# A recurrence followed by two MLPs on one core: later weight loads, two inverses one behind the other, and identity products in TensorE's waits

## What is computed

```python
for t in range(S):
    y[:, :, t] = np.einsum('bhd,bhde->bhe', rt, state)
    Sa = np.einsum('bhde,bhe->bhd', state, at)
    state_decay = state * wt[:, :, None, :] - np.einsum('bhd,bhe->bhde', Sa, bt)
    state = state_decay + np.einsum('bhd,bhe->bhde', vt, kt)
...
h = x @ w_in                                   # 320 x 2048
x = np.maximum(0.01 * h, h) @ w_out            # 2048 x 320
gate = 1.0 / (1.0 + np.exp(-(x @ w_gate)))     # 320 x 1536
out = (gate * (x @ w_val)) @ w_out2            # 1536 x 320
```

## Time and profile before

| | us |
|---|---|
| median of three runs | 1167.99 |
| lowest and highest | 1159.88, 1174.42 |
| the profiled execution | 1176.43 |
| its span, first to last instruction | 1174.7 |

### The profile page before, as it was taken

How to read it: one execution, slowest core, us unless ns; L and a number is a source line. 1 busy time by engine, 2 the same in 40 slices (tenths; PEclk the granted TensorE clock), 3 DMA queues, 4 the chain that set the end, 5 groups by cost and what they waited for, 6 DMA issues and landing times.

```text
span 1174.7 us, 35939 instructions
## 1 busy us (share of the span) xinstructions
PE 1061.2 (90%) x15840; PEld 905.7 (77%) x15840; DVE 596.3 (51%) x1307; ACT 397.6 (34%) x782; POOL 109.4 (9%) x100
## 2 busy tenths in 40 slices
PE   3476595888999999989999999999999999999998
PEld 3476474776878787877778787888888888888887
DVE  8674674796667865666756232443323232322322
ACT  2323232333443533343344334553322222222322
POOL 7201102022020202020200000000000000000000
PEclk9996698988999998989999999999999999999999
DMA  5836215536353533444351205330010102020000
GB/s 174 260 70 217 57 29 142 130 93 172 85 139 87 165 84 107 114 131 94 105 140 51 70 8 170 102 93 23 15 45 1 59 1 59 1 59 1 23 1 23
DMA packets 134985, 99.79 MB, mean 85 GB/s; under 512 B 96560, under 2 KB 111920, under 8 KB 134832
## 3 DMA queue, kind: packets, MB, share of 16 engines
q1 hardware_dynamic: 132384, 85.06, 27.2%
q0 software_dynamic: 2448, 12.45, 3.0%
HBM read 78.61 MB, written 18.87 MB: 83 GB/s over the span
## 4 chain that ended last, share of the span: by engine, by line
PE 75%; DVE 9%; issue 8%; DMA 3%; ACT 2%; POOL 1%; SPq 1%; ACTq 0%; DVEq 0%; POOLq 0%
PE pair_low L866 12%; PE pair L919 11%; PE pair_low L919 6%; PE bank L919 6%; DVE prod L1402 3%; PE bank L939 3%; PE bank L938 3%; PE bank L937 3%; DVE t_unit L1406 2%; PE bank L840 2%; PE bank L831 2%; PE pair_low L883 2%; PE pair_low L884 1%; PE pair_low L885 1%; PE bank L883 1%
## 5 line engine op out<-in xcount | busy, mean ns | idle before, releaser
L1452 DVE TENSOR_TENSOR g_lo<-g_full,g_hi 128x512 fp32r<-128x512 f32 x168 | 122.7, 730 | 237.1 <-ACT g_hi L1167 237.0
L1167 ACT CAST g_hi<-g_full 128x512 fp32r<-128x512 f32 x168 | 104.4, 621 | 134.7 <-DVE g_full L1504 131.6
L866 PE MATMUL pair_low<-x_hi,w_up 128*128 128x512 f32 x440 | 131.8, 432 | 6.2 <-ACT x_hi L1176 3.4
L1160 ACT ACTIVATE g_full<-pair_low 128x512 f32<-128x512 f32 x88 | 52.7, 599 | 211.3 <-PE pair_low L866 198.6
L1402 DVE TENSOR_TENSOR prod<-t_unit,p_unit 128x126 f32<-128x126 f32 (+22 forms) x341 | 93.9, 275 | 24.8 <-DMA p_unit<-p_dram 14.6
L1406 DVE TENSOR_TENSOR t_unit<-t_unit,prod 128x126 f32<-128x126 f32 (+22 forms) x341 | 96.7, 284 | 11.7
L866 PEld LDWEIGHTS pair_low<-x_hi,w_up 128*128 128x128 f32 x440 | 82.3, 200 | 25.8 <-ACT x_hi L1176 3.5
L1504 DVE TENSOR_TENSOR g_full<-pair,h_sb 128x512 f32<-128x512 f32 x36 | 24.9, 691 | 112.8 <-PE pair L919 112.0
L866 PE MATMUL pair_low<-x_lo,w_up 128*128 128x512 f32 x264 | 78.4, 407 | 0.0
L1504 DVE TENSOR_TENSOR g_full<-bank,h_sb 128x512 f32<-128x512 f32 x36 | 24.9, 691 | 94.7 <-PE bank L919 86.3
L383 POOL TENSOR_TENSOR k_sb<-k_sb,inv 128x512 f32<-128x512 f32 x24 | 32.5, 1360 | 368.0 <-DMA k_sb<-in_kF 368.0
(11 more groups left out here) (232 smaller groups left out, 2564.4 us busy)
## 6 DMA issues: line engine op xcount, KB each, us to landing
b_sb<-in_bF SPq DMA_DIRECT2D x12, 512.0 KB, 6.3
a_sb<-in_aF SPq DMA_DIRECT2D x24, 256.0 KB, 6.4
k_sb<-in_kF SPq DMA_DIRECT2D x12, 512.0 KB, 5.0
v_sb<-in_vF SPq DMA_DIRECT2D x12, 512.0 KB, 6.7
r_sb<-in_rF SPq DMA_DIRECT2D x12, 512.0 KB, 8.6
p_unit<-p_dram SPq DMA_DIRECT2D x22, 256.0 KB, 4.1
w_raw<-in_wF SPq DMA_DIRECT2D x20, 260.0 KB, 3.6
stage<-in_w_out POOLq DMA_DIRECT2D x7, 640.0 KB, 7.2
```

The costliest lines, as they stand in the source:

```text
L866: last = nc.tensor.matmul(up_bank(m)[:], lhs, rhs, start=(e == 0), stop=(e == len(products) - 1))
L1160: nc.scalar.activation(g_full[:], up_bank(m)[:], ACT.Lrelu).then_inc(g_ready, 1)
L1167: nc.scalar.copy(g_hi[:, m % 2], g_full[:]).then_inc(g_hi_ready, 1)
L1452: nc.vector.tensor_tensor(g_lo[:, m % 2], g_full[:], g_hi[:, m % 2].bitcast(F32), ALU.subtract).then_inc(g_lo_ready, 1)
```

## The change

Five things are changed, all in the start and in stages of unit 2.

1. POOL asks for the first weights after T of unit 0 has landed (`t_loaded` at 64) and no longer after P of unit 0 has; its b, a and k of units 0, 1 and 2 all stand ahead of the weights, and k 0 and 1 behind b and a of halves 2 and 3.
2. DVE does the scans of halves 0 to 5 first, then the inverses of units 0 and 1 one behind the other. The masked copies `ka` 0 to 3, which stood between scans and inverses, now stand inside the inverses, behind column 18. To allow it, scans 0 to 2 have places for `inv` of their own (`spare_d`, laid over `w_dn1`), and raw decays of halves 4 and 5 use places of `w_first`.
3. `fill` puts products of the identity with itself (128 x 128) into TensorE's list: 24 at the beginning, 10 before the first `first`, and two or three at eight later places.
4. The state ahead of unit 0 is zero, so `sn` and `y_begin` of halves 0 and 1 are gone. `kb` 2 and 3 stand ahead of `first` 2 and 3, `kb` 4 and 5 inside the first MLP steps. ACT does `act_a` 4 and 5 behind `u` and `ut` of halves 0 and 1. Six columns of unit 2's inverse and two weight splits stand behind y of unit 0. Splits 1 to 3, which ACT did early, are done later.
5. `STEPS`: stage (2, 0) has five MLP steps where it had seven.

```diff
@@ START_ORDER, STEPS @@
-        STEPS = {(2, 0): [0, 1, 2, 3, 4, 5, 6], (2, 1): [7], (2, 2): [], (2, 3): [8], (2, 4): [], (2, 5): [],
+        STEPS = {(2, 0): [0, 1, 2, 3, 4], (2, 1): [5], (2, 2): [6], (2, 3): [7], (2, 4): [], (2, 5): [8],
...
@@ gpsimd_program @@
-            for n in range(2):
+            for n in range(4):
                 pool_b(pool, n)
                 pool_a(pool, n)
-            pool_k(pool, 0)
-            pool_k(pool, 1)
-            for n in range(2, 4):
-                pool_b(pool, n)
-                pool_a(pool, n)
-            pool.wait_ge(p_loaded[0], 32)
-            for i in range(4):
-                load_piece(pool, i)
-            pool_k(pool, 2)
-            pool_k(pool, 3)
+            for n in range(4):
+                pool_k(pool, n)
             for n in range(4, 6):
                 pool_b(pool, n)
                 pool_a(pool, n)
-            for i in range(4, 8):
+            pool.wait_ge(t_loaded, 64)
+            for i in range(8):
                 load_piece(pool, i)
...
@@ tensor_start @@
+            fill(pe, 24)
             pe_a_ka(pe, 0, None)
             pe_a_ka(pe, 1, None)
...
-            pe_sn(pe, 0)
-            pe_sn(pe, 1)
             pe_a_ka(pe, None, 2)
             pe_a_ka(pe, None, 3)
+            fill(pe, 10, "kb", 1)
             pe_first(pe, 0)
             pe_first(pe, 1)
+            fill(pe, 2, "kb", 1)
...
-            pe_y_begin(pe, 0)
-            pe_y_begin(pe, 1)
             pe_y_end(pe, 0)
             pe_y_end(pe, 1)
             pe_sn(pe, 2)
             pe_sn(pe, 3)
+            pe_kb(pe, 2)
+            pe_kb(pe, 3)
             pe_first(pe, 2)
             pe_first(pe, 3)
...
+        def fill(pe, count, op=None, n=0):
+
+            if op is not None:
+                emptied(pe, op, n)
+            free = bank[1] if op is None else bank[bank_of(op, n)]
+            for _ in range(count):
+                nc.tensor.matmul(free[:, 0:P], ident[:], ident[:], start=True, stop=True)
...
@@ scalar_start @@
-            act_a(act, 4)
-            act_a(act, 5)
             act_u(act, 0)
-            act_ut(act, 0)
             act_u(act, 1)
+            act_ut(act, 0)
             act_ut(act, 1)
+            act_a(act, 4)
+            act_a(act, 5)
...
@@ vector_start @@
-            for n in range(4):
+            for n in range(6):
                 dve_decay(dve, n)
+            inverse_first(dve, 0)
+            inverse_columns(dve, 0, 0, 18)
             dve_ka(dve, 0)
             dve_ka(dve, 1)
-            dve_decay(dve, 4)
-            inverse_first(dve, 0)
-            inverse_columns(dve, 0, 0, C - 1)
+            inverse_columns(dve, 0, 18, C - 1)
+            inverse_first(dve, 1)
+            inverse_columns(dve, 1, 0, 18)
             dve_ka(dve, 2)
             dve_ka(dve, 3)
-            dve_decay(dve, 5)
-            inverse_first(dve, 1)
-            inverse_columns(dve, 1, 0, C - 1)
+            inverse_columns(dve, 1, 18, C - 1)
...
@@ sync_program @@
             store_t(sp, 0)
             load_t(sp, 0)
-            load_w(sp, 6)
             store_p(sp, 4)
             store_p(sp, 5)
+            load_p(sp, 2)
+            load_a(sp, 6)
             store_t(sp, 1)
             load_t(sp, 1)
-            load_p(sp, 2)
-            load_a(sp, 6)
```

More of the change, by code:

```diff
@@ L67, in rwkv_mlp_kernel @@
         w_up3 = sb(ctx, "w_up3", [P, 5, GW], F32R)
+        w_dn1 = sb(ctx, "w_dn1", [P, GT, DN], F32R)
         w_up = [sb(ctx, f"w_up{i}", [P, 5, GW], F32R) for i in range(3)] + [w_up3]
-        w_dn = [sb(ctx, f"w_dn{i}", [P, GT, DN], F32R) for i in range(2)] + [w_dn2, w_dn3]
+        w_dn = [sb(ctx, "w_dn0", [P, GT, DN], F32R), w_dn1, w_dn2, w_dn3]
         x_f = sb(ctx, "x_f", [P, 3 * BLK])
@@ L840, in pe_y_end @@
                     last = nc.tensor.matmul(o[half(i, D), q * L:(q + 1) * L], kb_tok[:, c, i, q],
-                                            vrur(n, i)[:, q], start=False, stop=(q == TQ - 1), skip_group_check=True)
+                                            vrur(n, i)[:, q], start=(n < 2 and q == 0), stop=(q == TQ - 1),
+                                            skip_group_check=True)
             last.then_inc(bank_filled[bank_of("y", n)], 1)
@@ L969, in tensor_start @@
             pe_ut_u(pe, 1)
+            fill(pe, 3, "first", 0)
             pe_st(pe, 0)
@@ L1019, in tensor_program @@
                             down_products(pe, m - 1)
[L1020 to L1021 removed]
+                        if (g, s, m) == (START, 0, 1):
+                            pe_a_ka(pe, 6, None)
+                        if (g, s, m) == (START, 0, 2):
+                            pe_kb(pe, 4)
+                            pe_kb(pe, 5)
+                        if (g, s, m) == (START, 0, 3):
+                            pe_a_ka(pe, 7, None)
                     if s == 0 and now:
@@ L1133, in act_sn @@
             filled(act, "sn", n)
-            multiplied(act, "y", n - 1 if n >= 2 * START else n - 2)
+            if n >= 2 * START:
+                multiplied(act, "y", n - 1)
             bk = bank_of("sn", n)
@@ L1251, in scalar_start @@
             act_rhs(act, 1)
-            act_sn(act, 0)
-            act_sn(act, 1)
-            for i in range(4):
-                split_hi(act, i)
             act_first(act, 0)
@@ L1274, in scalar_start @@
             act_cross(act, 3)
-            act_kb(act, 2)
-            act_kb(act, 3)
             act_u(act, 2)
+            act_u(act, 3)
             act_ut(act, 2)
-            act_u(act, 3)
             act_ut(act, 3)
-            for i in range(4, 8):
+            for i in range(2, 8):
                 split_hi(act, i)
-            act_kb(act, 4)
-            act_kb(act, 5)
             act_x(act, 0)
@@ L1293, in scalar_program @@
                         act_g(act, m)
-                        if (g, s) == (START, 0) and m in (2, 5):
-                            act_a(act, 6 + m // 5)
+                        if (g, s, m) == (START, 0, 2):
+                            act_a(act, 6)
+                        if (g, s, m) == (START, 0, 3):
+                            act_kb(act, 4)
+                            act_kb(act, 5)
+                        if (g, s, m) == (START, 0, 4):
+                            act_a(act, 7)
                     if (g, s) == (START, 0):
@@ L1525, in vector_start @@
             dve_y(dve, 1)
-            for i in range(4):
-                split_lo(dve, i)
+            inverse_first(dve, 2)
+            split_lo(dve, 0)
+            inverse_columns(dve, 2, 0, 6)
+            split_lo(dve, 1)
             dve_st(dve, 2)
```

78 lines of the change are left out of this document (44 added, 34 removed), and 17 rows, old and new, of tables (START_BANKS, START_ORDER).

## The result

The changed kernel takes 1174.11 us (median of 20 runs, 1168.36 to 1181.26); the kernel before takes 1167.01 (20 runs, 1159.88 to 1174.42). The ratio is 1.0058, 95% interval 1.0038 to 1.0078. The forecast was about 1159, 9 us faster; it is 7 us **slower**, 1 us outside the range, and still within 2%. The profiled execution of after (the changed kernel) took 1175.24 and lies near its median; that of before (1176.43) lies above all 20 of its timed runs, so spans are not compared, only times up to the first MLP product.

What follows compares the result with a forecast made beforehand. TensorE was taken as the bound from 300 us, with a chain of waits ahead of it. The MLP starting 6.3 us earlier plus 3.0 in unit 2 gave -9.3, a median of about 1159 us, range 1146 to 1173.

Steps and rivals of the forecast that it cites:

- Scans, inverses, POOL: DVE's start: inverse 0 from 30.2 to 54.8 us, six POOL operations costing 5.3, inverse 1 ending at 74.1.
- first at 54.8 + 7.8 = 62.6: Unit 0: its first product runs at 62.6 us, 7.8 after inverse 0 ends, for T's store, load and wait.
- T of unit 1 is late next: SP's queue: T of unit 1 stored near 85.2 us, against 77.34 before; first 2 at 93, bounds 88 and 97.
- T of unit 1 queues behind P of unit 2: Rival, chance 0.17: SP's queue puts first 2 at 98 and the MLP at 143; slower, 1170 us.
- What is won behind it: Unit 1 after first 2: ut 4.4 us later, near 97.4; state product at 102 us against 107.61.
- From st 2 to the last y took 15.6: Unit 1's end: 15.6 us before, less part of the clock, plus 1.1 for identity products; y ends at 116.5.
- I take 18.0: Last y of unit 1 to the MLP: 18.0 us for 17.55, bounds 16.5 and 20; MLP begins at 134.5.
- Unit 2 ... I take 3 won: Wait for T at first 4 and fewer MLP steps in unit 2: 3 us won, bounds 6 and -2.
- The chain warms and nothing queues: Rival, chance 0.18: identity products keep 2.4 GHz, POOL costs 2, v_nu lands in 6; time 1147 us.
- Nothing moves: Rival, chance 0.08: T of unit 2 and the state chain of units 2 and 3 set the time; 1167 us.

Runs made afterwards that it cites:

- e2: The changed kernel with masked copies ka 2 and 3 between the inverses of units 0 and 1, not behind column 18 of unit 1; median 1169.7 us.
- e5: The changed kernel with both edits, T of unit 1 earlier in SP's list and ka 2 and 3 between the inverses; 0.9982 against the kernel before.
- e1: The changed kernel with store and load of T of unit 1 ahead of store_p 4, 5, load_p(2) and load_a(6) in SP's list; 1.0021 against before.
- e3: The changed kernel without any identity product, their waits kept; 1.0073 against the kernel before.
- e8: e5 without any identity product, their waits kept; 0.9994 against the kernel before.
- e7: e5 with the STEPS table and spread of inverse columns of before, seven MLP steps in stage (2, 0); 0.9999 against the kernel before.
- e9: The kernel before, with POOL asking for all weights behind T of unit 0 and b, a and k of units 0 to 2; 0.78% slower than before.
- e6: e5 with weight splits 2 and 3 earlier, on ACT behind kb 3 and on DVE behind split 1; its time is that of e5.
- e10: e1 with scan 5 and ka 2 and 3 between the two inverses; ratio not given, first 2 came 4.9 us earlier than in e5.
- e12: e11 with scan 5 between the inverses and v, r and v_nu of unit 1 asked for ahead of P of unit 2; 0.9900 against before.
- e13: e12 with weight pieces 6 and 7 asked for only once first 3 has been multiplied; 0.9898 against the kernel before.
- e11: e5 with six of the eight weight splits moved into waits of ACT and DVE; ratio not given, last y to first MLP product 11.4 us.
- e4: The changed kernel with the first four weight pieces asked for at about 31 us; 3 us slower than the changed kernel, intervals overlapping.

## Why the prediction was wrong

**Scans, inverses, POOL: right.** Inverse 0 began at 30.99 (30.2), ended at 55.32 (54.8), inverse 1 at 74.43 (74.1). Six DVE instructions took 1.11 to 1.24 us beside six POOL ones; against neighbours of 0.23 to 0.28 that is a loss of 5.4, and the whole inverse took 24.3 against 19.0 for inverse 1, which had no POOL operation beside it. Forecast: 5.3. The rule of the Trainium skill (SBUF — State Buffer, Who interferes with whom), taken whole, gave 7.1; the trace agrees with it in kind, one slow DVE instruction for each POOL operation, and has less, since a held-up instruction lasted 1.11 to 1.24 us in all, its own 0.23 to 0.28 among them.

**"first at 54.8 + 7.8 = 62.6": failed, 66.75.** The time of T was right (e2: 62.85). The step left out that `first` waits for a bank as well, and for DVE's copy of `ka` 2, which the diff moved into inverse 1. The prediction mentioned that copy, as 0.69 us of DVE time, and didn't ask who waits for it. That moved st 0 (80.96 for 76.2; 76.6 in e2) and all behind it, and is worth about 4 us by e5 against e1 (0.9982 and 1.0021).

**"T of unit 1 is late next": the right mechanism, too small.** The store was put at 85.2, it came at 91.49. 4.3 of these 6.3 us are the bank's (87.16 in e2); the other 2.0 are the forecast's own error (`load_p(2)` went out at 85.31 in e2, where the forecast had 83.5). From the store to the load took 5.3 for 4.4, and from there to `first` 6.5 for 4.1. By then weight traffic ran (DMA share 0.97 from 98 to 103.3 us): T took a median of 2.5 us from issue to landing in before, and in after

```profile
DMA to landing us min/median/max: 2.0/5.1/5.2
```

`first` 2 came at 103.38 for 93. The rival "T of unit 1 queues behind P of unit 2" was to decide from `first` 2 at 97 with the MLP at 143; e2, in which only the bank is repaired, has 97.37 and 142.81, and a median of 1169.7 for the rival's 1170. The forecast had 11 us between ready and stored, e2 has 13, after 17: the wait was seen, and taken to be paid for by what stands behind it.

**"What is won behind it": failed.** 9 us were put from `first` 2 to st 2; after took 15.79, e5 14.67, and before took 16.89. The first part of it, `first` 2 to `ut`, was put at 4.4 us. It took 8.2 in after, 7.6 in e5 and 6.7 to 8.7 in all eleven kernels with the identity products, but 4.2 in e3 and 4.5 in e8, which have none; in e8 `first` 2 came at 94.11 and

```profile
98.64 0.33 PE L792 MATMUL pair<-t_sb,rhs_sb 64*40 64x64 f32 x2
```

So the 4.4 was right without them, and what the forecast left out is the price of the five that stand there (two and three, 2.87 us in after). It did count eight in three places, but from st 2 to the last y; in `tensor_start` these eight stand between `first` 2 and st 2, where they took 4.5 us in all, and only three stand behind st 2. (The list has seven later places of such products in all, not the eight that the section on the change gives.) The second part, `ut` to st 2, was put at 4.6 and took 7.6 in after, with the last three of the eight (1.65) and a gap of PE without a releaser in it (2.70 at 116.59); before, with such a gap of 3.01 in it, took 7.0.

**"From st 2 to the last y took 15.6", taken as 14.5:** 9.63 in after, at a clock near 1 (0.96). This gave back 4.9, and by luck: e7, with the same products, took 16.7. **"I take 18.0" for the tail:** 19.91, within its bounds; the tail is 17.54 in e9 with four splits behind the last y as before had them, 19.9 to 20.2 with the changed kernel's six (nine kernels), 14.0 in e6 with four, whose pieces were asked for early, and 11.4 to 11.9 with two.

The sum for the first product: +10.4 (`first` 2), +6.8, -4.9, +1.9, that is 14.2 on 134.5, the 148.71 of the trace.

**"Unit 2 ... I take 3 won": not seen.** `first` 4 stood 37.05 behind the first product for 38.5 in before, and waited 8.73 us for T. From the first product to the end (the median of the runs less its start in the one trace) it is 1025.4 in after and 1026.2 in before, 0.8 won, less than runs scatter.

**The rivals.** "The chain warms and nothing queues" is excluded: T of unit 1 queued for 17 us, and the clock was 0.56 from 40 to 80 us. "Nothing moves" is excluded by what comes next. That time follows the first MLP product about one to one, on which the sum rested, held throughout: while its start went from 132.4 to 149.4 us, the median less that start stayed between 1023.9 and 1029.9 in all kernels. (Within the traced executions themselves it is 1019.9 to 1029.0, and 1035.6 in the slow one of before.)

## What to carry to other kernels

An operation moved later in one engine's list keeps all who wait for its result, and all who need the buffer or bank that it empties: write down both before costing the move, and look up in the queue what stands between "ready" and "sent". A load moved later has to take its consumers along, since the first of them in an in-order list holds up what stands behind it. Where chains end close together, one repair shows only the next wait (`first` 2 came 4.9 us earlier in e10 and the time did not fall), so follow each run's trace to what is late next and repair that too. And before a few us between two traces are put down to an edit, look for two kernels whose lists are the same up to that point, as e5 and e7 are, and see how far they differ.

## What the runs showed of the hardware

**The granted clock that a profile shows can be wrong until it first changes.** e3 and e5 do the same products from 20 to 45 us. The window of e3, whose records show 1.00 up to 80 us:

```profile
20.00:45.00 25.00, 13.82 (x353) 13.20 (x356) 23.04 (x56) 5.24 (x14) 9.31 (x6) 1.00 0.55 150
```

and that of e5, which has 24 identity products at the beginning and shows a fall of the clock behind them:

```profile
20.00:45.00 25.00, 13.79 (x352) 13.17 (x355) 23.17 (x52) 5.01 (x13) 11.40 (x8) 0.50 0.61 176
```

Busy 13.82 and 13.79 us: the clock was the same, half. So the mean clock of the whole span, 0.956 in before and 0.940 in after, says nothing of a slower chip in after; that stretch is recorded in one and not in the other (e3, after without the products, shows 0.961).

**Gaps of PE without a releaser.** "issue" in brackets does not mean that nothing was waited for: `first` 0 waits for T in e2 and has it too (8.93). But inside the products of `kb` 3, which have no wait between them, most traces have a gap, and it stands at a fixed product: of the 64 rows of L710 for `kb` 2 and 3, seven lie behind it in each of e12, e13, e6, e7, e5, e11, e4 and after; in before, e9 and e3, which have no identity products ahead, 30 do. So the gap belongs to a place in PE's list of instructions. Its length differs. It was 3.95 us in before, 4.89 in e9, 3.12 in e6, 6.86 in e12 and 3.50 in e13, at DMA shares of 0.97 to 1.06; it was 2.02 in e4 and 2.03 in after, at shares of 0.04 and 0.19, and 1.48 in e7 at a share of 1.00. Full DMA engines go with the long gaps but do not make every gap long. The page has a queue of instruction loads,

```profile
q8 instruction: 125, 2.05, 0.8%
```

16 KB each, and in the traces one of them began inside each of these five gaps of 3 us and more (at 96.16 in e12) and inside none of the shorter ones of `kb` 3, though a longer gap catches one more easily by chance. That PE waits at such a place for its own instructions, behind the weights, fits all this, but no run took the instruction load itself away: it is argued, not shown.
